# Joining three pairs of loads in a queue-bound linear-attention and soft-MoE kernel

## The reference

```python
kv = np.einsum('bhsd,bhse->bhde', k, v)            # 8 batches, 8 heads, 576 tokens, 64
out = np.einsum('bhsd,bhde->bhse', q, kv)
rms = np.sqrt(np.mean(out * out, axis=-1, keepdims=True) + 1e-06)
x = (out / rms * g_norm)                           # then (4608, 512)
logits = x @ phi                                   # (4608, 32): 8 experts, 4 slots each
d = softmax of logits over the tokens; slot_input = d.T @ x
slot_out[e] = np.maximum(slot_input[e] @ w1[e], 0) @ w2[e]     # 512 -> 1024 -> 512
c = softmax of logits over the slots; result = c @ slot_out
```

## Time and profile before

| | |
|---|---|
| median of three runs | 172.03 us (171.95 to 172.06) |
| the profiled execution | 171.93 us |
| its span, first to last instruction | 170.6 us |
| TensorE busy, weight loads busy | 148.2 us, 100.6 us |
| VectorE, ScalarE, GpSimd busy | 87.4 us, 88.8 us, 59.4 us |
| DMA, all queues | 71.63 MB, mean 420 GB/s |
| HBM read, written | 61.94 MB, 9.44 MB |

### The profile page before, as it was taken

How to read it: one execution, slowest core, us unless ns; L and a number is a source line. 1 busy time by engine, 2 the same in 40 slices (tenths; PEclk the granted TensorE clock), 3 DMA queues, 4 the chain that set the end, 5 groups by cost and what they waited for, 6 DMA issues and landing times.

```text
span 170.6 us, 3976 instructions
## 1 busy us (share of the span) xinstructions
PE 148.2 (87%) x1704; PEld 100.6 (59%) x1704; DVE 87.4 (51%) x187; ACT 88.8 (52%) x230; POOL 59.4 (35%) x73
## 2 busy tenths in 40 slices
PE   7989699899899899999988999899969889989200
PEld 3469578799679787887885673333326543445000
DVE  1122159583677464857266998526886036318300
ACT  3036587787956888869498870204131045218300
POOL 7000707777456476382736589000000004000000
PEclk9999999999999999999999999999999999999755
DMA  5999999999999999999999899999899999999996
GB/s 184 419 421 424 440 421 438 471 423 444 458 412 423 432 441 447 454 399 454 442 423 454 380 473 414 423 408 460 366 423 434 446 434 401 424 418 422 439 447 259
DMA packets 3843, 71.63 MB, mean 420 GB/s; under 512 B 778, under 2 KB 778, under 8 KB 913
## 3 DMA queue, kind: packets, MB, share of 16 engines
q1 hardware_dynamic: 3425, 71.20, 97.7%
q0 software_dynamic: 400, 0.18, 0.4%
HBM read 61.94 MB, written 9.44 MB: 418 GB/s over the span
## 4 chain that ended last, share of the span: by engine, by line
PE 49%; DMA 29%; ACT 11%; DVE 3%; SPq 2%; issue 1%
PE psum L93 49%; DMA arena<-in_w_dram 15%; DMA arena<-in_kv_dram 14%; ACT arena L93 3%; ACT bd L93 3%; ACT sq L93 2%; SPq L93 2%; ACT part L93 1%; DVE ms L93 1%; ACT r L93 1%; ACT d L93 1%; DVE logits L93 1%; DVE d L93 0%; DVE part L93 0%; DVE arena L93 0%
## 5 line engine op out<-in xcount | busy, mean ns | idle before, releaser
L93 PE MATMUL psum<-bd,arena 128*128 128x192 f32 (+1 forms) x320 | 54.8, 335 | 2.8 <-ACT bd L93 1.6
L93 PEld LDWEIGHTS psum<-bd,arena 128*128 128x128 f32 (+1 forms) x320 | 45.2, 179 | 8.4 <-ACT bd L93 2.8
L93 PE MATMUL psum<-arena 128*64 128x64 f32 (+2 forms) x896 | 36.3, 270 | 1.9 <-DMA arena<-in_kv_dram 1.0
L93 PEld LDWEIGHTS psum<-arena 128*64 128x64 f32 (+2 forms) x896 | 27.5, 129 | 14.6 <-issue 4.8
L93 DVE TENSOR_REDUCE ms<-sq 128x16 f32<-128x1024 f32 (+1 forms) x19 | 22.1, 1163 | 26.5 <-ACT sq L93 26.0
L93 POOL TENSOR_TENSOR arena<-arena,r 128x512 f32<-128x512 f32 x34 | 34.7, 1042 | 0.0
L93 POOL TENSOR_TENSOR part<-part,r 128x512 f32<-128x512 f32 x17 | 17.8, 1048 | 47.9 <-DVE r L93 47.9
L93 ACT COPY arena<-psum 128x512 f32<-128x512 f32 (+2 forms) x48 | 30.7, 649 | 6.0 <-PE psum L93 5.9
L93 ACT ACTIVATE sq<-psum 128x512 f32<-128x512 f32 x36 | 21.5, 597 | 9.6 <-PE psum L93 9.2
L93 ACT COPY part<-psum 128x256 f32<-128x256 f32 (+1 forms) x38 | 13.6, 359 | 12.6 <-DVE part L93 11.4
L93 DVE TENSOR_REDUCE logits<-part 128x64 f32<-128x512 f32 (+1 forms) x18 | 17.8, 991 | 0.1
(11 more groups left out here) (77 smaller groups left out, 110.0 us busy)
## 6 DMA issues: line engine op xcount, KB each, us to landing
arena<-in_w_dram SPq DMA_DIRECT2D x2, 8064.0 KB, 30.2
arena<-in_t_dram SPq DMA_DIRECT2D x1, 6912.0 KB, 37.5
arena<-in_w_dram SPq DMA_DIRECT2D x1, 6400.0 KB, 23.0
arena<-in_w_dram SPq DMA_DIRECT2D x3, 2048.0 KB, 19.2
arena<-in_kv_dram SPq DMA_DIRECT2D x2, 2304.0 KB, 23.7
arena<-in_kv_dram SPq DMA_DIRECT2D x1, 4608.0 KB, 42.8
arena<-in_w_dram SPq DMA_DIRECT2D x1, 4096.0 KB, 25.8
arena<-in_kv_dram SPq DMA_DIRECT2D x1, 3584.0 KB, 32.4
```

What stands on the lines that cost most here:

```text
L93: self.inst, self.token = method(*args, **kwargs), None
```

## The change

Batch 1 becomes one load instead of two, and all its steps stand ahead of T=4. The first part of q of batches 2 and 3 moves from a load of its own into batch 3's load, which waits for `kv.read`; for that the places of q and of batch 4 move down by 16 blocks. Units 3 and 4 of w2 become one load, after `pair_h(0)` as before; `load_w(4)` and `load_w(5)` are then what 5 and 6 were. Six products of zeros go ahead of expert 4's first half, in a pair of banks taken from the ring.

```diff
-LATE_FILL = (4, 3, 3, 1, 1)
+LATE_FILL = (4, 3, 3, 1, 1, 6)
-KV_AT = (0, 106, 124, 0, 52, 70, 106, 124)
-Q_AT = (142, 34, 88, 142)
+KV_AT = (0, 106, 124, 0, 36, 70, 106, 124)
+Q_AT = (142, 18, 88, 142)
...
-    (0, blocks(("w2", 3, 0, 16))), (16, blocks(("w2", 4, 0, 16))),
+    (0, blocks(("w2", 3, 0, 16), ("w2", 4, 0, 16))),
...
-    kv_landed[1, 0] = load_row(KV_AT[1], kv_in[1, :, :2304])
-    kv_landed[1, 1] = load_row(KV_AT[1] + 9, kv_in[1, :, 2304:])
+    kv_landed[1, 0] = kv_landed[1, 1] = load_row(KV_AT[1], kv_in[1])
     q_landed[0, 1] = load_row(Q_AT[0] + 8, q0_in[:, 2048:])
     kv_landed[2, 0] = kv_landed[2, 1] = load_row(KV_AT[2], kv_in[2])
-    q_landed[1, 0] = load_row(Q_AT[1], q1_in)
...
-    kv_steps.update({(1, -2): (0,), (1, -1): (1, 2)})
+    kv_steps[1, 0] = 0, 1, 2
...
-    def fill(t, n, cols=512):
+    def fill(t, n, cols=512, after=()):
...
-                after=[zeros_set],
+                after=[zeros_set, *after],
...
-    kv_landed[3, 0] = kv_landed[3, 1] = load_row(KV_AT[3], kv_in[3], after=[kv.read])
+    kv_landed[3, 0] = kv_landed[3, 1] = q_landed[1, 0] = load_row(KV_AT[3], kv3_in, after=[kv.read])
...
     load_w(3, [h_read[0]])
-    load_w(4, [h_read[0]])
     combine(0)
     pair_h(1)
-    load_w(5, [h_read[1]])
+    load_w(4, [h_read[1]])
...
     pair_h(2)
-    load_w(6, [h_read[2]])
+    load_w(5, [h_read[2]])
...
     expert_y(1, 1)
+    bank, t, free = pairs.take()
+    fill(t[:, 0], LATE_FILL[5], after=[free])
+    pairs.freed[bank] = pe.done()
     for e in range(4, NE):
         y_made = expert_y(e, 0)
```

More of the change, by code:

```diff
@@ L132, in first_pieces, with soft_moe_linear_attention @@
         at += n * size
-def soft_moe_linear_attention(nc, first_in, kv_in, q0_in, q1_in, kv4_in, kv5_in, t3_in, w_in, out):
+def soft_moe_linear_attention(nc, first_in, kv_in, q0_in, kv3_in, kv4_in, kv5_in, t3_in, w_in, out):
     pe, dve, act, pool = (
@@ L1167, in build_program @@
     shapes = {
-        "first": (P, HEAD + 2304), "kv": (4, P, TOK), "q0": (P, TOK), "q1": (P, 2048),
+        "first": (P, HEAD + 2304), "kv": (3, P, TOK), "q0": (P, TOK), "kv3": (P, TOK + 2048),
         "kv4": (P, 2560 + TOK), "kv5": (P, 2 * TOK), "t3": (P, 3 * TOK),
@@ L1215 @@
         "in_first_dram": first,
-        "in_kv_dram": kv[:4],
+        "in_kv_dram": kv[:3],
         "in_q0_dram": qm[0],
-        "in_q1_dram": np.ascontiguousarray(qm[1][:, :2048]),
+        "in_kv3_dram": np.concatenate([kv[3], qm[1][:, :2048]], axis=1),
         "in_kv4_dram": np.concatenate([qm[1][:, 2048:], kv[4]], axis=1),
```

## The result

The changed kernel takes 172.71 us (172.28 to 172.78, 8 runs) against 171.83 us (171.57 to 172.07) for the kernel before beside it: ratio 1.0047, 95% interval 1.0038 to 1.0056, so slower by 0.65 to 0.96 us. The prediction said 171.8 us, range 171.35 to 172.4. Its profiled execution took 172.78 us.

What follows compares the result with a forecast made beforehand. The prediction took the sum of packets on the slowest engine of SyncE's DMA queue to bound the kernel. It summed -0.21 us for three joins and nothing for the rest to 171.8 us, range 171.35 to 172.4.

Steps and rivals of the forecast that it cites:

- the margin at the last store: Kernel's end: the last store waits for the queue, with 0.8 to 3.5 us to spare after its issue.
- Part 1, the price of a join: SyncE's queue: each join saves eight row prices of 8.6 ns per engine, 0.07 us; three joins 0.21 us.
- Parts 2 and 3: First phase: batch 1's later step and q's wait delay TensorE by about 1.2 us together, taken up at 125.42; nothing charged.
- The wait at T=9: TensorE's T=9, at 33.76 before, now waits for q in batch 3's load until 34.9, about 1.2 us.
- Part 4, the first mix: Joined units 3 and 4 make the first mix 1.5 us later; zeros covered by the wait; nothing charged.
- The first half's stores stand behind unit 7 in the queue and don't matter.: After the first mix: the first half's stores, 1.5 us later, add nothing to the time.
- The 0.55 us of idle weight side at 144.74 would absorb delay.: TensorE's idle 0.55 and 0.53 us would cut the 1.5 us delay to 0.4 us for the second half.
- the prediction's signs of being wrong: Last store starting under 2.7 us after issue, clock under 1.00 before 157, or free DMA slices around 80 to 110.
- B: Last store issued too late, through TensorE's clock if the zeros don't hold it: 172.5 to 175.2 us; chance 0.14.
- A: Each join also saves a pause at a transfer's end, up to 0.42 us more: 171.4 us; chance 0.14.
- C: The join does nothing, the row's price being an artefact or lost again: 172.0 us, within 0.2%; chance 0.17.

Runs made afterwards that it cites:

- late_mix1: Kernel before with five zero products between experts 6 and 7 of the second half only: 171.87 us, 1.0006.
- the cover: A 768 KB load nobody reads, queued right behind unit 7; added to the kernel before 173.66 us, to the changed kernel 173.44 us.
- w_only: Kernel before with units 3 and 4 of w2 joined and the six zeros, nothing else: 172.61 us, 1.0045.
- late_small: Kernel before with all eight small stores of the first half (SyncE's and GpSimd's, with its step) issued one output piece later: 172.65 us, 1.0054.
- kv_only: Changed kernel with units 3 and 4 in two loads again and no zeros, leaving two joins: 171.61 us, 0.9988; a second time 171.70 us, 0.9990.
- the three zeros: Kernel before with three zero products ahead of expert 7 in the first half: 172.13 us, 1.0017.
- cover_late12: Kernel before with the extra 768 KB load behind unit 7 and twelve zero products ahead of expert 7: 174.05 us, 1.0131.
- late_mix0: Kernel before with six zero products between experts 6 and 7 of the first half, all loads unchanged: 172.48 us, 1.0036.
- late_sync: Kernel before with only SyncE's small stores issued one output piece later, GpSimd's at their times: 172.30 us, 1.0032.
- twelve zeros: Kernel before with twelve zero products ahead of expert 7 in the first half: 173.24 us, 1.0087.
- cover_before: Kernel before with one more 768 KB load, read by nobody, queued right behind unit 7: 173.66 us, 1.0104.
- cover_late: Kernel before with the extra 768 KB load behind unit 7 and six zero products ahead of expert 7: 173.53 us, 1.0099.

## Why the prediction was wrong

**The queue bounds the kernel, and the margin at the last store.** Right. late_mix1 moved the last store's issue by 0.8 us and not the end.

**Part 1, the price of a join.** Right in size: two joins gave 0.17 to 0.21 us (forecast 0.14), and under the cover three joins gave 0.2 us (173.66 to 173.44; forecast 0.21), though the intervals are about as wide as these gains, and wider in the second case. The Trainium skill, "DMA: Bandwidth & Descriptors", section "Anatomy of one DMA", has about 2.0 us of fixed cost per DMA. The runs don't show it for transfers that queue behind each other, where two joins gave 0.2 us.

**Parts 2 and 3.** Right. The wait at T=9 was there (1.23 us) and was taken up at 125.

**Part 4, the first mix.** Right up to 138.34. The working after it failed twice:
- *"The first half's stores stand behind unit 7 in the queue and don't matter."* This is the step that failed. I had the times of unit 7 only as landings, and these are the slowest engine's. The Trainium skill, "DMA: Bandwidth & Descriptors", section "Why a DMA increments its semaphore by 16 and not by 1", says why that is not the time of all: "a DMA runs on up to 16 SDMA engines that finish independently, and the semaphore counts them". In the kernel before, the small stores begin to run at 145.6, four microseconds ahead of unit 7's landing (the packets under 8 KB in the next view). The last of them was issued at 144.0, and by the prediction's own bound up to 2.7 us pass between issue and start, so there was little slack. The change issues all of them 1.3 us later, while the first engine reports unit 7 at 146.0 in both kernels. What this cost is w_only's 0.8 us and late_small's 0.9 us, where the prediction had nothing.
- *The 0.55 us of idle weight side at 144.74 would absorb delay.* It stayed. The second such idle took up only 0.3 us: y of the second half was 1.05 us late, not 0.4. By late_mix1, where a last store 0.8 us late cost nothing, this was wrong without consequence.

None of the prediction's signs of being wrong showed. The last store of the changed kernel lands at 171.4, so by its 7.3 us of rows it starts 3.3 us after its issue, and the granted clock is 1.00 from 24 to 157. The signs watched the last store, the clock and the middle of the kernel; none watched the small stores.

The kernel before, DMA in 145.6 to 146.0 us:

```profile
DMA packets 18, 0.19 MB, mean 486 GB/s; under 512 B 3, under 2 KB 3, under 8 KB 8
q1 hardware_dynamic: 15, 0.18, 103.2%
q0 software_dynamic: 3, 0.02, 11.0%
```

The changed kernel, the same stretch:

```profile
DMA packets 16, 0.12 MB, mean 297 GB/s; under 512 B 5, under 2 KB 5, under 8 KB 11
q1 hardware_dynamic: 14, 0.11, 63.1%
q0 software_dynamic: 2, 0.01, 29.4%
```

**The rivals.** B had the right sign and began at the right place, the late first half, but named the wrong reason (the clock; it stayed at 1.00) and the wrong store (the last; it is the small ones). The clock's half of B was true of the version without zeros. A, a pause saved at each transfer's end, isn't needed for what two joins gave. C was wrong. My chance of 0.14 for slower was too low for a stretch in which three waits had to absorb a delay.

**What stays open.** The busy share by a view's window is a poor witness. In 145 to 147 us it is 88% in the changed kernel and 94% with the small stores late, but 99% in the kernel with six zeros, which loses too, 96% with the late second half, which loses nothing, and 92% in kv_only, the fastest of all. The finer count in 146 to 147 does better: 0.3 to 1.9 engine-us of idleness in every run that loses 0.5 us or more uncovered, at most 0.1 in those that lose nothing and in all with the cover. It misses the 0.3 us of the three zeros and the 0.4 us of cover_late12.

Even 1.4 engine-us are only 0.1 us for each of 16 engines. They can make 0.9 us only if they fall on few, and the reports of the last store show just that. In the kernel before, all 16 engines report it by 170.57. In the changed kernel 14 do so by 170.72 and two at 171.28 and 171.42. In w_only, late_mix0, late_small and late_sync, too, all but one or two report by 170.7, the others between 171.0 and 171.6. The end follows one or two engines that lost their turn. How much of their lateness is idleness and how much are slow packets, as below, the runs don't part. The profile doesn't name a packet's engine, so I can't say which engines they are.

## What to carry to other kernels

Where loads give way to stores in one queue, ask whether the first stores are there when the *first* engine finishes the last load. A landing time is the slowest engine's, here 3.5 us later. Joining loads saved little where they queued anyway (two joins 0.2 us of 172), and what a join delays must be followed to the stores, not just to the next wait. A cheap test for such a place is a load that nobody reads, queued ahead of it. If a delay costs nothing any more once that load is there, the queue was running empty.

## What I had not expected of the hardware

Single packets of a small store took several times their usual time in the runs where the small stores came late. In 145.6 to 146.0 the two 6144-byte packets of GpSimd's queue took 29.4% x 16 x 0.4 / 2 = 0.94 us each in the changed kernel, and 11.0% x 16 x 0.4 / 3 = 0.23 us each before (the views above). By the trace's packets, each run has 29 of this size, nearly all at 0.23 us. The longest took 0.8 us in late_small and late_sync, 0.9 to 1.0 in w_only and late_mix0, 1.3 with twelve zeros and 0.7 in cover_late12. In the runs that lose nothing none passes 0.56 us, and in kv_only, cover_before and cover_late all took the usual time. One packet of 0.94 us on the engine that ends last would be 0.7 us of the 0.9 us by which the span grew; whether it was there isn't recorded.
